# Sixteen split-weight slots of a fused attention and two-layer kernel, each begun 16 bytes further on

## The reference

```python
x = attention(q, k, v, proj)             # 1536 x 512
h = x @ moe_w_in                         # 512 -> 2048
g = where(h >= 1, h, where(h <= -1, 0, (h + 1) ** 2 / 4))
x = g @ moe_w_out                        # 2048 -> 512
h = x @ moe2_w_in
out = (h - tanh(h)) @ moe2_w_out
```

## Time and profile before

| | |
|---|---|
| median of three runs | 781.04 us |
| the profiled execution | 781.19 us |
| its span, first to last instruction | 779.2 us |
| TensorE busy | 756.5 us (97%) |
| VectorE, ScalarE, GpSimd busy | 436.3, 355.2, 321.9 us |
| mean granted TensorE clock | 0.996 of full speed |

### The profile page before, as it was taken

How to read it: one execution, slowest core, us unless ns; L and a number is a source line. 1 busy time by engine, 2 the same in 40 slices (tenths; PEclk the granted TensorE clock), 3 DMA queues, 4 the chain that set the end, 5 groups by cost and what they waited for, 6 DMA issues and landing times.

```text
span 779.2 us, 11744 instructions
## 1 busy us (share of the span) xinstructions
PE 756.5 (97%) x3712; PEld 637.0 (82%) x3712; DVE 436.3 (56%) x757; ACT 355.2 (46%) x701; POOL 321.9 (41%) x267
## 2 busy tenths in 40 slices
PE   4999999999999999999999999999999999999998
PEld 2788888888888888888888888888888888888886
DVE  1999999999997565335343577763222321222213
ACT  2889889889886333334233333342212222121212
POOL 4789889889899996000000165660000000000000
PEclk8999999999999999999999999999999999999999
DMA  5533523523222333000000032220000100010001
GB/s 195 178 111 107 163 76 107 163 76 107 82 81 68 127 131 109 0 1 1 0 1 1 0 109 89 100 82 1 0 1 1 54 0 0 0 54 1 1 0 55
DMA packets 17871, 47.35 MB, mean 61 GB/s; under 512 B 2289, under 2 KB 4465, under 8 KB 17841
## 3 DMA queue, kind: packets, MB, share of 16 engines
q1 hardware_dynamic: 17840, 46.94, 18.6%
HBM read 38.87 MB, written 3.15 MB: 54 GB/s over the span
## 4 chain that ended last, share of the span: by engine, by line
PE 73%; DVE 9%; issue 5%; POOL 5%; ACT 4%; DMA 2%; SPq 1%; DVEq 0%; POOLq 0%; ACTq 0%
PE ps L575 28%; PE ps L498 28%; PE ps L475 5%; DVE g_raw L815 5%; PE ps L489 5%; PE ps L461 2%; PE ps L464 2%; PE ps L432 2%; POOL probs L355 2%; DVE g_mid L812 1%; POOL k_b L340 1%; ACT g_mid L697 1%; ACT g_hi L703 1%; ACT probs L621 1%; DMA k_raw<-kk 1%
## 5 line engine op out<-in xcount | busy, mean ns | idle before, releaser
L498 PE MATMUL ps<-x_hi,w 128*128 128x512 f32 (+1 forms) x768 | 252.1, 390 | 0.0
L823 DVE TENSOR_TENSOR g_lo<-g_raw,g_hi 128x512 fp32r<-128x512 f32 x96 | 70.2, 731 | 244.6 <-ACT g_hi L703 244.6
L703 ACT ACTIVATE g_hi<-g_raw 128x512 fp32r<-128x512 f32 x96 | 60.7, 632 | 289.8 <-PE ps L575 228.0
L498 PEld LDWEIGHTS ps<-x_hi,w 128*128 128x128 f32 x768 | 144.1, 188 | 29.6
L498 PE MATMUL ps<-x_lo,w 128*128 128x512 f32 (+1 forms) x384 | 149.4, 389 | 0.0
L575 PE MATMUL ps<-g_hi,w 128*128 128x512 f32 x384 | 125.9, 389 | 0.3 <-DVE g_lo L823 0.3
L575 PE MATMUL ps<-w,g_hi 128*128 128x512 f32 x384 | 118.3, 389 | 0.0
L312 POOL TENSOR_SCALAR w<-stage 128x1024 fp32r<-128x1024 f32 x32 | 38.2, 1194 | 166.9 <-PE ps L575 165.7
L753 DVE TENSOR_TENSOR p_lo<-ps,p_hi 128x384 fp32r<-128x384 f32 x192 | 97.9, 551 | 9.6 <-ACT p_hi L631 7.8
L355 POOL TENSOR_SCALAR probs<-probs,row_inv 128x768 f32<-128x768 f32 x96 | 86.9, 909 | 23.4 <-DVE row_inv L747 23.4
L631 ACT ACTIVATE p_hi<-ps 128x384 fp32r<-128x384 f32 x192 | 84.7, 489 | 24.5 <-PE ps L475 22.5
(11 more groups left out here) (48 smaller groups left out, 902.8 us busy)
## 6 DMA issues: line engine op xcount, KB each, us to landing
stage<-weights SPq DMA_DIRECT2D x32, 512.0 KB, 3.3
qk_raw<-qk SPq DMA_DIRECT2D x16, 384.0 KB, 3.5
q_raw<-qq SPq DMA_DIRECT2D x16, 384.0 KB, 3.1
k_raw<-kk SPq DMA_DIRECT2D x16, 384.0 KB, 3.8
q_a<-q_b SPq DMA_DIRECT2D x16, 192.0 KB
v_raw<-v SPq DMA_DIRECT2D x16, 192.0 KB, 2.4
out<-stage SPq DMA_DIRECT2D x12, 256.0 KB, 2.1
q_b<-bits SPq DMA_DIRECT2D x16, 54.0 KB
```

The lines of the kernel that those rows point to most:

```text
L498: last = nc.tensor.matmul(ps[:, f % H_BANKS, :], w[:, f, wp, k * P:(k + 1) * P], xs[:, k, bass.ds(t * TOK, TOK)], start=(k == 0 and wp == ...
L703: nc.scalar.activation(g_hi[:, slot, :], g_raw[:, slot, :], ACT.Copy).then_inc(g_hi_ready, 1)
L823: nc.vector.tensor_tensor(g_lo[:, slot, :], g_raw[:, slot, :], g_hi[:, slot, :].bitcast(F32), ALU.subtract).then_inc(g_split, 1)
```

## The change

The stride from one slot of `w` to the next grows by four numbers (`SKEW`, 16 bytes), from 8192 to 8208 bytes. So slot `f` begins 16 `f` bytes further on than before, counted within 256 bytes: slot 0 where it was, slot 1 16 bytes further, and slot 15 240 bytes further. Within a slot nothing moves: the high half and the low half stay 4096 bytes apart, and each slice of 128 or 512 numbers stays contiguous. The whole tile is padded to 512 bytes more than before, and `w_place` grows by 512 bytes, so that every other tile behind `w` and behind `w_place` moves by 512 bytes and keeps its offset within 512 bytes. No instruction is added, removed or moved, and no shape changes.

```diff
@@ -43,6 +43,7 @@
 LINE = 128
+SKEW = 4
@@ -106,7 +107,7 @@
-            sb("w_place", [P, PRE, 2, CH], F32R, att)
+            sb("w_place", [P, PRE * 2 * CH + LINE], F32R, att)
@@ -131,7 +132,9 @@
-        w = sb("w", [P, FC, 2, CH], F32R)
+        w_slots = sb("w", [P, FC * (2 * CH + SKEW) + FC * SKEW], F32R)
+        w = w_slots[:, 0:FC * (2 * CH + SKEW)].rearrange("p (f r) -> p f r", f=FC)[:, :, 0:2 * CH]\
+            .rearrange("p f (i c) -> p f i c", i=2)
```

## The result

The changed kernel takes 792.67 us, the median of four runs (792.2 to 793.2), beside 781.02 for the kernel before. The ratio is 1.0147 with a 95% interval of 1.0135 to 1.0159. It is slower by 11.65 us, and my range ended at 784.8.

The account below looks back on a forecast made before the run. The prediction took TensorE's back-to-back matmuls, 226.7 ns apart, to bound the kernel. Its three terms, 0 + 0 + 0 against the profiled 781.19 us (0.15 above the median), gave 781.1 us, range 780.2 to 784.8.

Parts of the forecast that it names:

- First step: Tiles behind `w_place` and `w` move by 512 bytes: taken as 0, bounds 0.9 us to either side, in attention.
- Second step: TensorE's loads and streams of 15 of 16 slots shift by 16 to 240 bytes: 0; bounds 23.3 us gain, 14.4 loss.
- A load has room ... Cost 0: TensorE's shifted loads in both layers: a load could become 0.11 us longer before the stream waits, so 0.
- the bit products: Nearest row for a shift: weights differing by 32 bytes within 256, all loads 143 ns, all matmuls 486; read as 0.
- one more piece per stream: Loss bound for second-layer `project` streaming `w`: 0.9 to 14.4 us; with a 64-byte piece, 3.6 us.
- The argument against the collision: TensorE's load and stream: a stream passes the load's position whichever offset it began at, so skew moves meetings without removing them.
- Third step: GpSimd's shifted writes of `w` and the subtraction's read: covered by TensorE's pace, 0; bounds -0.3 and +2.1 us.
- A: TensorE's load-stream collision is real, skew ends it: 757.8 us, partial form 775; chance 0.06 in full, 0.07 in part.
- B: A shifted stream is slower, in second-layer `project`: 3.6 us, 784.7 in all; chance 0.09.
- C: GpSimd's shifted writes are slower: up to a factor of 1.3, 2.1 us, 783.2 in all; chance 0.06.
- D: The 512-byte move alters attention by up to 0.9 us either way, 780.2 to 782.0; within no change's 0.72.

Follow-up runs that it names:

- the history run: Matmuls alone, layers, attention and result left out: stretches of 96 with the load 16 bytes on, entered from 0, 8 and 64; 226.7 or 233.3 ns a matmul.

## Why the prediction was wrong

**What bounds the kernel** was right: TensorE's 2304 matmuls follow each other without a gap, and only their spacing, or a wait, could move the time. It was the spacing. One reading in it was wrong: the chain is not TensorE's alone from 257 us on. From 436 to 519 us, in the last token tile of the first layer, it runs through the gate, with rows such as

```profile
450.37 2.66 DVE g_raw L815
```

That cost nothing here, because TensorE's groups take 2.72 us beside it, with the one wait of 0.3 us; and when they grew, the same additions came 5.6 us apart in place of 5.4.

**First step, the move by 512 bytes: right.** 0 was forecast, 0.9997 was measured.

**Second step, TensorE's reads: wrong, and it is the whole error.** It was put at 0 for loads and 0 for streams, and measured 11.4 us: from one matmul of the layers to the next it took 231.8 ns in the mean, against 226.8 before. "A load has room ... Cost 0" held the load for a thing of its own that is slow or fast and hides beside the stream. A load isn't longer now (188 ns before and after); the pair of load and stream is slower. The room of 0.11 us was no cover, since what is lost is lost in the stream. The row taken as the nearest, the bit products, was the wrong neighbour: they are float32, and float32 showed no dependence on the six offsets tried. I noted "at a slower stream" and still took its 0. And the loss was bounded as "one more piece per stream", 3.6 us in the likely form, when the loads of the first layer pay just as much.

**The argument against the collision** drew the wrong end from a sound start. "A skew moves the meetings, it doesn't remove them" is near what was found, but I let it speak for no change. I had also written that all pairs in the trace have the same offset within 256 bytes and that the uniform 226.7 ns is therefore no refutation. That cuts both ways: a place that the whole trace occupies says nothing of its neighbours, for better or for worse, and I gave the worse no chance in this form. One row of before might have warned me. This is its chain at the change from the first token tile to the second, where `g_lo` was ready only 0.26 us ahead of `project` (353.12 and 353.38 us), so that its first load couldn't come early:

```profile
353.54 2.77 PE ps L575 x12
356.31 2.72 PE ps L498 x12
```

The group takes 2.77, the starts of its first ten matmuls 224 to 237 ns apart, much as in the disturbed stretches, and then 227 and 226. The 226.7 ns were a state into which load and stream settle, not a constant of the matmul.

**Third step, GpSimd: right.** Medians of 1048 and 2400 ns against 1060 and 2397, and the matmuls lose the same with GpSimd idle.

**The rivals.** A (the collision ends) had the right object, a load that meets a stream, with the wrong sign. The rule of the Trainium skill that I had set against it, page "TensorE: Matmul & The Clock Gate", section "What happens when you issue a matmul", says that loading the next weights takes nothing from the running stream because the two have ports of their own. By that rule the time would have stayed at 781. The runs disagree for float32r, and agree for bfloat16 and float32. The 2.5 ns over the columns that the same page states, section "Wait — 56ns, not 53.3ns?", are met by bfloat16 (215.8 against 215.7 ns) and missed by float32r by 11. B (a shifted stream) had the right sign and the wrong mechanism, as the first layer and the kernel moved as a whole show. C and D didn't occur.

What I said would show it did: a group between 306 and 350 us that differs from 2.72.

**What stays open.** That the loss comes from load and stream placed against each other is shown; the rhythm itself is not explained. Several settled spacings are multiples of 16 cycles of 2.4 GHz (416, 544, 560; 272 and 288 for 256 columns), others are not (548, 552), the pattern has a period of 256 bytes, and it depends on what went before. That would fit two readers that block each other in some interleaved memory and fall into step, but this is a guess: no run looked inside, and the two simple rules for the excess (R1 and R2) and the bare distance all failed. Nor was a placement found that is faster than that of the kernel before: none of the 64 load offsets and 16 stream offsets tried beat 226.7 ns for 512 columns.

## What to carry to other kernels

With float32r matmuls of 512 columns back to back, place the loaded and the streamed operands so that they begin at the same offset within 256 bytes, a multiple of 32, and pad tiles to multiples of 256; here that is worth 11 of 781 us. Another placement, such as a load 16 bytes on, can seem harmless in a short test and cost 3% of each matmul once something has disturbed the rhythm. For shorter streams measure first: at 256 columns a load 64 bytes off was faster than one at 0, and at 448 columns the load at 0 was among the slowest. When every row of a trace shows the same value under the same condition, it says nothing about another condition: before calling an address change free, ask which distances the trace has never seen. And when two neighbours could be the nearest row, take the one with the same number format and rate.

## What the runs showed of the hardware that I had not expected

- A float32r matmul of 512 columns took 226.7 ns in the settled state and 228 to 239 outside it in the mean of a stretch, on an otherwise idle core; bfloat16 took 215.8 and float32 2 x 429.2 at each of six load offsets.
- The state has memory: the same operands gave 226.7 or 233.3 ns for 96 matmuls on end.
- The second to the twelfth matmul of the history run started 427 ns apart, although their stretch shows a granted clock of 1.00, the level of 2.4 GHz (10 matmuls in 4.00 us, against 76 in 17.00 later). 512 columns at the lower level, 1.2 GHz, would be 426.7 ns with nothing over. Whether these matmuls ran at that level isn't shown; if they did, the excess of 13.3 ns isn't there at it. TensorE was idle until 8.99 us:

```profile
9.00:13.00 4.00, 4.00 (x10) 3.13 (x11) 0.00 (x0) 0.00 (x0) 1.00 1.01 382
30.00:47.00 17.00, 17.00 (x76) 14.08 (x75) 0.00 (x0) 0.00 (x0) 1.00 0.00 0
```
